# Sorted-order second mixture: x2, its logits and its dispatch kept in the order of the first mixture's groups

## The chip, the cores and the metric

The kernel runs on one core of a Trainium2 chip. The metric is the device time of one launch in microseconds (us).

## What is computed

Three stages follow each other. A linear-attention recurrence over 4 x 8 heads, 768 steps and 48 channels gives 3072 tokens of 384 numbers. The first mixture passes a token through one of 8 experts (384 to 1024 to 384) only if a score is positive; the others go on unchanged. The second, soft mixture needs all tokens: 32 slots are weighted sums over all tokens, 8 experts work on 4 slots each, and each token's output is a weighted sum of the 32 slot outputs.

```python
skip_score = x @ w_skip
do_compute = skip_score > 0
out = x.copy()
xc = x[do_compute]
logits = xc @ w_gate
e_idx = np.argmax(logits, axis=1)
...
for e in range(E):
    mask = e_idx == e
    h = np.maximum(xc[mask] @ w1[e], 0.0)
    y[mask] = gate_w[mask, None] * (h @ w2[e])
out[do_compute] = xc + y
...
logits = x @ phi
d = np.exp(logits - logits.max(0)); d /= d.sum(0) + 1e-09
slot_input = d.T @ x
...
c = np.exp(logits - logits.max(1)); c /= c.sum(1) + 1e-09
return c @ slot_out
```

## The kernel before

All five engines have their own hand-written instruction streams, joined by semaphores. P = 128 partitions; x is held as 24 tiles of 128 tokens x 384 (`x_sb`), all float32.

**Attention and gate** (up to about 165 us). 16 pairs of heads; then each tile is turned on TensorE (`gate_tiles`, L548), its scores are computed (`gate_scores`, L560) and turned back. The x tiles go to DRAM (`tokens`, L406), and zeros are written over `results` (L397).

**Routing front.** VectorE (L1116 to L1180) picks each token's expert, ranks the tokens with two products on TensorE (L603, L604), and builds one-hot tables. 24 narrow products (L611) invert them into lists: `take_i`, the token row for each place in sorted order, and `put_i`, where it goes back. TensorE runs filler products meanwhile (`idle_products`, L595: 8, 20, then 2 ahead of each of 8 register loads).

**First mixture.** The taken tokens stand sorted by expert, each expert padded to sub-tiles of 32; four sub-tiles are a group of 128 rows, and here there are 13 groups. GpSimd gathers the rows of a group with an indirect DMA (L1328) into `rows_in`. VectorE turns them (`turn_rows`, L1183); VectorE and ScalarE each copy half of a sub-tile's x (`take_x`, L1187 and L908); TensorE runs `first_layer` (L620) of the next sub-tile and then `second_layer` (L628) of this one; ScalarE applies relu (L917), VectorE turns the hidden values (L1194), ScalarE evicts the result (L936, L937) and VectorE adds its two halves (L1226). After four sub-tiles GpSimd scatters the 128 result rows to `results` (L1333). SyncE loads each next expert's weights as they come free, and the first slot experts' weights (L409 to L427).

**Collection.** When the last scatter has landed, SyncE reads `results` back in token order (L431). VectorE computes x2 = result x weight + x for 24 tiles (L1247), while TensorE turns them in six batches of four tiles (L690) and computes their logits (`slot_scores`, L672); 42 filler products (L670) stand ahead. The logits are exponentiated in two halves, each against its own maximum, turned, and used as dispatch weights (`dispatch`, L706); the halves are merged by rescaling (L1261 to L1272).

**Slot experts and output.** `slot_hidden` (L744) and `slot_back` (L759) run over 8 experts, whose weights SyncE loads into places as they come free (L433 to L447). Between them the comb weights (softmax over the slots) are turned (L777, L786) from logits that stayed in SBUF. After the fold (L792, L793) 24 output tiles are computed (L802), scaled by ScalarE and VectorE (L1006, L1292) and written in twelve DMAs (L451).

## Time and profile before

| | us |
|---|---|
| runs of the kernel | 400.13, 398.88, 398.15 (median 398.88) |
| the profiled execution | 398.49, clock granted on average 0.981 |
| its span, first to last instruction | 396.7 |
| busy: PE, weight load, DVE, ACT, POOL | 364.4, 278.1, 276.1, 219.6, 103.6 |
| data moved | 105.90 MB, mean 267 GB/s |

In the rows PE is TensorE, PEld its weight loads, DVE VectorE, ACT ScalarE, POOL GpSimd and SPq the queue of SyncE. A "x" counts instructions (a float32 product counts as two). In timelines an entry merges neighbouring instructions of one line; the bracket at its end is the idle time of the engine before it and what ended it. Times are from the span's start. PEclk is the granted TensorE clock as a share of 2.4 GHz.

### The profile page before, as it was taken

The numbers are of one execution on the slowest core, as the hardware profiler recorded it, in microseconds if no ns is written. First come the engines' busy times: TensorE is split into PE (matmuls) and PEld (weight loads), VectorE is DVE, ScalarE is ACT, GpSimd is POOL, SyncE is SP. The second block draws the span as 40 slices with busy tenths as digits, with TensorE's granted clock in tenths as the row PEclk, the third lists the DMA queues.
The fourth block names the chain that finished last, engine by engine and source line by source line (L and its number), as shares of the span: only waits on it lengthen the run. The fifth ranks groups of instructions, "written<-read, shape, count | busy, mean of one in ns | idle before, by whom it ended". The sixth has DMA issues, their size and how long they took to land.

```text
span 396.7 us, 14472 instructions
## 1 busy us (share of the span) xinstructions
PE 364.4 (92%) x5811; PEld 278.1 (70%) x5811; DVE 276.1 (70%) x557; ACT 219.6 (55%) x682; POOL 103.6 (26%) x136
## 2 busy tenths in 40 slices
PE   0799999999999999899999999999999999999980
PEld 0578877777777788787777777777777778855350
DVE  8999999999999934574666666666666654932051
ACT  1468777777677774304565565556565542841141
POOL 2222444334444360012322232222132330010000
PEclk9969999999999999999999999999999999999997
DMA  8956765567767999602195799696868817999839
GB/s 315 414 197 228 267 251 212 191 215 226 256 235 234 340 415 415 272 2 62 36 324 216 264 348 403 234 357 222 339 232 326 315 63 275 409 405 378 306 119 358
DMA packets 33432, 105.90 MB, mean 267 GB/s; under 512 B 3456, under 2 KB 14976, under 8 KB 31856
## 3 DMA queue, kind: packets, MB, share of 16 engines
q1 hardware_dynamic: 31536, 99.62, 67.7%
q0 software_dynamic: 1856, 5.70, 4.0%
q8 instruction: 30, 0.49, 0.5%
q14 instruction: 10, 0.08, 0.1%
HBM read 88.21 MB, written 17.10 MB: 265 GB/s over the span
## 4 chain that ended last, share of the span: by engine, by line
PE 55%; DVE 6%; DMA 2%; issue 1%; ACT 1%; SPq 0%; DVEq 0%; ACTq 0%; POOLq 0%
PE a_bank L624 18%; PE y_bank L633 17%; PE y_bank L749 3%; PE a_bank L765 3%; PE a_bank L557 2%; PE a_bank L690 2%; DVE x_sb L1292 1%; PE a_bank L597 1%; DMA back<-results 1%; PE y_bank L679 1%; PE y_bank L520 1%; PE a_bank L710 1%; DMA results<-work,put_now 1%; DVE k_in L1041 1%; PE y_bank L515 1%
## 5 line engine op out<-in xcount | busy, mean ns | idle before, releaser
L633 PE MATMUL y_bank<-w_sb,work 128*32 128x192 f32 x1664 | 78.5, 326 | 0.7 <-ACT work L937 0.7
L624 PE MATMUL a_bank<-w_sb,batch_t 128*32 128x256 f32 x1248 | 77.9, 381 | 0.0
L1315 POOL TENSOR_SCALAR_AFFINE_SELECT a_sb<-a_sb 128x512 f32<-128x512 f32 x48 | 51.3, 1071 | 85.6 <-ACT a_sb L837 85.6
L633 PEld LDWEIGHTS y_bank<-w_sb,work 128*32 128x32 f32 x1664 | 63.6, 110 | 10.8 <-DVE work L1194 3.4
L624 PEld LDWEIGHTS a_bank<-w_sb,batch_t 128*32 128x32 f32 x1248 | 42.2, 109 | 24.7 <-issue 11.0
L911 ACT ACTIVATE batch_t<-work 32x96 f32<-32x96 f32 x108 | 30.4, 281 | 45.3 <-PE a_bank L624 32.1
L1194 DVE STREAM_TRANSPOSE work<-hid 128x256 f32<-128x256 f32 x53 | 23.3, 440 | 35.2 <-PE y_bank L633 32.8
L847 ACT ACTIVATE bonus_v<-v_sb,bonus 128x48 f32<-128x48 f32 x192 | 44.9, 327 | 0.0
L494 PE MATMUL a_bank<-r_in,k_in 64*128 64x128 f32 x384 | 36.7, 313 | 1.2 <-DVE r_in L1042 0.3
L494 PEld LDWEIGHTS a_bank<-r_in,k_in 64*128 64x128 f32 x384 | 27.1, 200 | 11.5 <-issue 6.7
L1226 DVE TENSOR_TENSOR ys<-work 32x192 f32<-32x192 f32 x78 | 27.2, 348 | 8.7 <-ACT work L937 6.6
L936 ACT ACTIVATE work<-y_bank 64x192 f32<-64x192 f32 x52 | 16.8, 324 | 23.2 <-PE y_bank L633 22.9
L1019 DVE TENSOR_TENSOR_SCAN decay<-wrk_sb,ones_at 128x780 f32<-128x780 f32 x16 | 28.4, 1778 | 1.2
L1028 DVE TENSOR_TENSOR_SCAN decay<-wrk_sb,inv_at 128x780 f32<-128x780 f32 x16 | 28.7, 1795 | 0.1
L837 ACT ACTIVATE a_sb<-a_bank 128x512 f32<-128x512 f32 x48 | 28.4, 592 | 0.6 <-PE a_bank L494 0.6
L1189 DVE COPY batch_t<-work 32x96 f32<-32x96 f32 x108 | 26.4, 245 | 2.7 <-PE a_bank L624 0.4
L515 PE MATMUL y_bank<-r_in,state 64*48 64x128 f32 x320 | 21.4, 276 | 3.9 <-DVE x_sb L1055 3.9
L520 PE MATMUL y_bank<-a_sb,v_sb 128*48 128x128 f32 x384 | 24.3, 276 | 0.0
L1333 POOL DMA_INDIRECT results<-work,put_now x14 | 14.6, 1041 | 34.5 <-DVE work L1226 33.6
L515 PEld LDWEIGHTS y_bank<-r_in,state 64*48 64x48 f32 x320 | 18.2, 160 | 6.4 <-issue 5.9
L464 PE MATMUL ktok_bank<-ident,k_in 128*128 128x128 f32 x64 | 10.8, 293 | 12.9 <-DVE k_in L1041 12.9
L597 PE MATMUL a_bank<-ident 128*128 128x128 f32 x172 | 22.0, 290 | 0.4 <-DVE take_i L1170 0.3
(245 smaller groups left out, 569.2 us busy)
## 6 DMA issues: line engine op xcount, KB each, us to landing
w_sb<-in_moe_w SPq DMA_DIRECT2D x20, 1536.0 KB, 8.6
wrk_sb<-in_wrk SPq DMA_DIRECT2D x16, 768.0 KB, 7.6
e_sb<-in_moe_w SPq DMA_DIRECT2D x8, 1536.0 KB, 12.8
wrk_sb<-in_wrk SPq DMA_DIRECT2D x15, 780.0 KB
v_sb<-in_vt SPq DMA_DIRECT2D x16, 288.0 KB, 2.8
results<-work SPq DMA_DIRECT2D x1, 4608.0 KB, 15.2
tokens<-x_sb SPq DMA_DIRECT2D x4, 1152.0 KB, 23.0
x_sb<-in_moe_w SPq DMA_DIRECT2D x3, 1536.0 KB, 9.8
```

Of the source, the lines that this page charges most:

```text
L494: last = nc.tensor.matmul(a_bank[:, 2 * (g % 2) + a, (c % 2) * C:(c % 2 + 1) * C], k_in[rows, cols], r_in[n % 3][rows, cols], start=True, ...
L515: nc.tensor.matmul(y_cols[64 * a:64 * a + D, c * C:(c + 1) * C], state[n % 2][rows, :, c - 1], r_in[n % 3][rows, c * C:(c + 1) * C], start ...
L520: last = nc.tensor.matmul(y_cols[64 * a:64 * a + D, c * C:(c + 1) * C], v_sb[n % 4][:, c, a, :], a_sb[n % 2][:, a, c, :], start=False, sto ...
L624: last = nc.tensor.matmul(out[SUB * g:SUB * (g + 1), 0:FB], x[:, kk, :], w1_sb[j][:, kk, FB * g:FB * (g + 1)], start=(kk == 0), stop=(kk = ...
L633: last = nc.tensor.matmul(bank[4][SUB * g:SUB * (g + 1), 0:YW], h_t[:, SUB * k:SUB * (k + 1)], w2_sb[j][:, k, d:d + YW], start=(b == 0), s ...
L837: nc.scalar.activation(a_sb[n % 2][:, :, 2 * s:2 * s + 2, :].rearrange("p a c t -> p a (c t)"), a_bank[:, 2 * (g % 2):2 * (g % 2) + 2, 0:2 ...
L847: last = nc.scalar.activation(bonus_v[n % 2][:, c, a, :], v_sb[n % 4][:, c, a, :], ACT.Copy, scale=bonus[:, c, a:a + 1])
L911: last = nc.scalar.activation(x[SUB * o:SUB * (o + 1), :, :], turned[SUB * s:SUB * (s + 1), :].rearrange("p (k o t) -> p k o t", o=PER, t= ...
L1019: V.tensor_tensor_scan(decay[:, 0:SCAN], wrk_sb[i][:, 0:SCAN], ones_at[:, :], 0.0, ALU.mult, ALU.add).then_inc(mid_up_ready, 1)
L1028: V.tensor_tensor_scan(decay[:, SCAN:2 * SCAN], wrk_sb[i][:, SCAN:2 * SCAN], inv_at[:, :], 0.0, ALU.mult, ALU.add).then_inc(mid_down_ready, 1)
L1226: last = V.tensor_tensor(place_of[SUB * s:SUB * (s + 1), YW * d:YW * (d + 1)], y_low[rows, :], y_high[rows, :], ALU.add)
L1315: nc.gpsimd.affine_select(out=x, in_=x, compare_op=ALU.is_gt, fill=0.0, base=0, pattern=[[0, 2], [0, 2], [1, C]], channel_multiplier=-1).t ...
```

## The change

- `x_all` has 28 tiles, and `x_sb` is its last 24. The first mixture's result is no longer scattered: x2 of a group is made in SBUF, in sorted order, in `x_all[:, g]`. GpSimd copies the gathered rows there, gathers 128 gate weights from DRAM (`weights`), and adds the scaled results of the first 96 rows; VectorE adds the last 32.
- The tokens that skip the first mixture are dealt with ahead of the loop: phi logits of all 24 tiles come from the gate's turned tiles (six `gate_x` buffers instead of three), a mask product adds -1e30 for taken tokens, and all 24 tiles of `x_sb` are dispatched into bank 7 before the experts start.
- After the loop only the sorted tiles are turned: three batches of four, and a loop over the late batches, whose trip count is a register (at least 1; one for 13 groups). A mask from DRAM hides padding rows. Then 12 + 14 tiles are dispatched into two banks, and three parts are merged.
- Comb weights of the skipping tokens are stored to `combs[0]` in token order before the loop; those of sorted rows (32 numbers a row) are scattered by GpSimd to `combs[0]` and `combs[1]` in turn, and both are read back and added ahead of the last turn, which now stands behind the slot experts.
- All filler products go, and so do the fill of `results` with zeros over 4.6 MB (0.4 MB of `combs[1]` are cleared instead), the store and the reload of `results`. The slot experts' weights get other places and other waits.

The diff, cut to its core:

```diff
@@ SyncE @@
+            sp.wait_ge(weight_ready, 1)
+            with nc.allow_non_contiguous_dma(reason="a row of weights per partition"):
+                sp.dma_start(by_partition(weights), weight[:, :].unsqueeze(2)).then_inc(weight_stored, 16)
+            sp.wait_ge(mask_copied, 2)
+            sp.dma_start(masks, mask_bt).then_inc(tables_stored, 16)
+
+            sp.wait_ge(tables_stored, 16)
+            for i in range(BATCH):
+                sp.dma_start(mask_rows[NS * i:NS * (i + 1), :, :],
+                             masks.rearrange("(q i) t -> i q t", i=BATCH)[i:i + 1].to_broadcast([NS, XQ, P])).then_inc(ld_masks, 16)
+
+            sp.wait_ge(combs_a_ready, 1)
+            sp.dma_start(by_partition(combs[0])[:, 0:NT, :], comb[:, :, :]).then_inc(tables_stored, 16)
+
             sp.wait_ge(routed, 1)
-            groups = sp.value_load(tiles_i[0:1, E + 1:E + 2], min_val=1, max_val=MAX_GROUPS)
...
-            sp.wait_ge(results_stored, over)
-
-            for q in range(NT // 2):
-                sp.dma_start(back_rows(2 * q)[:, 2 * q % RING:2 * q % RING + 2, :],
-                             by_partition(results)[:, 2 * q:2 * q + 2, :]).then_inc(ld_rows[q], 16)
-            sp.wait_ge(x2_ready, RING)
+            sp.wait_ge(weigh_turned, 3)
+            load_e1(sp, 6)
+            sp.wait_ge(slot_parts_full, 2)
             load_e1(sp, 5)
-            sp.wait_ge(x2_ready, 2 * RING)
-            load_e1(sp, 4)
-            sp.wait_ge(x2_ready, NT)
-            load_e1(sp, 6)
-            sp.wait_ge(slot_parts_full, 1)
+            sp.wait_ge(slot_parts_full, 3)
             load_e1(sp, 7)
-            sp.wait_ge(slot_parts_full, 2)
             load_e2(sp, 4)
-            load_e2(sp, 5)
-            sp.wait_ge(slot_hidden_full, 1)
-            load_e2(sp, 6)
-            sp.wait_ge(slot_hidden_full, 2)
-            load_e2(sp, 7)
+            for e in range(5, E):
+                sp.wait_ge(slot_hidden_full, e - 4)
+                load_e2(sp, e)
+            sp.wait_ge(combs_all, 1)
+            for j, place in enumerate((comb[:, :, :], comb_odd)):
+                sp.dma_start(place, by_partition(combs[j])[:, 0:NT, :]).then_inc(ld_combs, 16)
...
@@ TensorE, front @@
+            for q in range(3):
+                phi_scores(q)
+            pe.wait_ge(pool_clear, 2)
+            nc.tensor.transpose(bank[7][0:NT, 3 * P:4 * P], mask_a[:, :], ident[:, :]).then_inc(mask_turned, 1)
+            phi_scores(3)
+            pe.wait_ge(mask_copied, 1)
+            for q in range(4):
+                mask_scores(q)
+            phi_scores(4)
+            phi_scores(5)
+            for q in range(4, NB):
+                mask_scores(q)
+            pe.wait_ge(logits_a_ready, 1)
+            turn(logit_t, logits_a_turned, 0, 4, bank[6])
+            pe.wait_ge(logits_a_ready, 2)
+            turn(logit_t, logits_a_turned, 4, NB, bank[4])
...
+            pe.wait_ge(weigh_ready, 1)
+            turn(weigh_t, weigh_turned, 0, 4, bank[0])
+            turn(weigh_t, weigh_turned, 4, NB, bank[1])
             pe.wait_ge(routed, 1)
+            pe.wait_ge(mask_b_ready, 1)
+            nc.tensor.transpose(bank[2][0:TILES, 0:P], mask_b[:, :], ident[:, :]).then_inc(mask_turned, 1)
             ends = [0]
+            pe.wait_ge(disp_ready, 1)
             for e in range(E):
-                idle_products(2)
+                n = NT * e // E
+                if n + NT // E > 16 >= n:
+                    pe.wait_ge(disp_ready, 2)
+                dispatch(n, n + NT // E, 0, NT, x_sb, bank[7])
                 ends.append(pe.value_load(tiles_i[0:1, e + 1:e + 2], min_val=1, max_val=MAX_GROUPS * PER))
+            pe.wait_ge(counts_ready, 2)
+            rest = pe.value_load(tiles_i[0:1, E + 2:E + 3], min_val=1, max_val=XQ - 3)
 
...
@@ TensorE, after the loop @@
+            x2_tiles(0)
+            x2_tiles(1)
+            early_scores(0)
+            x2_tiles(2)
+            early_scores(1)
+            pe.wait_ge(y_parts_ready, ends[E] + 1)
+            combs_turn(0, 0)
+            early_scores(2)
+            combs_turn(1, 1)
+            with pe.Fori(0, rest) as t:
+                pe.wait_ge(stage_ready, t + 1)
...
+                slot_scores(x_t4[1], bank[6], stage_turned)
+                pe.wait_ge(logit_t_ready, t + 4)
+                pe.wait_ge(combs_shifted, t + 2)
+                nc.tensor.transpose(bank[4][:, 3 * P:4 * P], logit_late[:, :], ident[:, :]).then_inc(combs_turned, 1)
+            pe.wait_ge(weigh_ready, 2)
+            turn(weigh_t, weigh_turned, 0, 3, bank[5])
+            pe.wait_ge(disp_ready, 3)
+            dispatch(0, 8, 0, B1, x_all, bank[0])
             pe.wait_ge(part_top_ready, 1)
-            nc.tensor.transpose(bank[0][0:1, 0:P], part_top[:, :], ident[:, :]).then_inc(tops_turned, 1)
-            pe.wait_ge(weigh_ready, 2)
-            turn(weigh_t, weigh_turned, HG, NB, bank[7])
-            dispatch(8, HG * BATCH)
+            nc.tensor.transpose(bank[2][0:1, 0:P], part_top[:, :], ident[:, :]).then_inc(tops_turned, 1)
+            combs_turn(2, rest + 2)
+            dispatch(8, B1, 0, B1, x_all, bank[0])
+            pe.wait_ge(weigh_ready, 3)
+            turn(weigh_t, weigh_turned, 3, XQ, bank[6])
             pe.wait_ge(top_row_ready, 1)
-            nc.tensor.matmul(bank[1][:, 0:1], top_row[:, :], ones[0:1, 0:1], start=True, stop=True).then_inc(tops_full, 1)
-            pe.wait_ge(disp_ready, 2)
-            dispatch(HG * BATCH, NT)
-
-            turn(logit_t, logits_turned, 0, 4, bank[6])
-            turn(logit_t, logits_turned, 4, NB, bank[7])
+            nc.tensor.matmul(bank[3][:, 0:1], top_row[:, :], ones[0:1, 0:1], start=True, stop=True).then_inc(tops_full, 1)
+            pe.wait_ge(disp_ready, 4)
+            dispatch(B1, MAX_GROUPS, B1, MAX_GROUPS, x_all, bank[1])
...
@@ VectorE, front @@
+            dve.wait_ge(logits_a_ready, 2)
+            V.tensor_reduce(less_part[:, 0:1], logit_t[:, 0:NB, :], AX.XY, ALU.max, negate=True).then_inc(less_a_ready, 1)
...
+            for j, n0, n1 in ((6, 0, 4 * BATCH), (4, 4 * BATCH, NT)):
+                dve.wait_ge(logits_a_turned, 1 if j == 6 else 2)
+                rows = bank[j][:, 0:(n1 - n0) * NS].rearrange("p (n s) -> p n s", s=NS)
+                link(V.tensor_reduce(top[:, n0:n1], rows, AX.X, ALU.max))
+                V.tensor_tensor(comb[:, n0:n1, :], rows, top[:, n0:n1].unsqueeze(2).to_broadcast([P, n1 - n0, NS]),
+                                ALU.subtract).then_inc(combs_a_shifted, 1)
...
@@ VectorE, end of a group @@
+                late = slice(TOK - SUB, TOK)
+                x2 = x_all[late, bass.ds(g, 1), :].rearrange("p o d -> p (o d)")
+                dve.wait_ge(ys_added, PER * g + PER + 1)
+                dve.wait_ge(ld_weight, 16 * g + 16)
+                dve.wait_ge(rows_kept, g + 1)
+                V.scalar_tensor_tensor(out=x2, in0=ys[late, :], scalar=weight_now[late, :], in1=x2,
+                                       op0=ALU.mult, op1=ALU.add).then_inc(x2_done, 1)
...
@@ VectorE, after the loop @@
+            dve.wait_ge(ld_masks, 64)
+            copy_tiles(0)
+            copy_tiles(1)
+            logits_of(0)
+            copy_tiles(2)
+            logits_of(1)
+            shift_combs(0, 1)
+            link(logits_of(2))
+            V.tensor_reduce(less_part[:, 1:2], group_top[:, 1:4], AX.X, ALU.max, negate=True).then_inc(less_part_ready, 1)
+            shift_combs(1, 2)
+            with dve.Fori(0, rest) as t:
...
+            dve.wait_ge(ld_combs, 32)
+            V.tensor_tensor(comb[:, :, :], comb[:, :, :], comb_odd, ALU.add).then_inc(combs_added, 1)
...
@@ ScalarE, after the loop @@
+            for q in range(3):
+                copy_tiles(q)
+            for q in range(2):
+                comb_exps(q, q + 1)
+            weigh(1, 0, 3)
+            with act.Fori(0, rest) as t:
+                for i in range(0, BATCH, 2):
+                    act.wait_ge(x2_transposed, BATCH * t + 3 * BATCH + i + 1)
+                    nc.scalar.activation(x_t4[1][:, :, i, :], bank[i][:, 0:DM].rearrange("p (k t) -> p k t", t=P),
+                                         ACT.Copy).then_inc(x2_copied_act, 1)
+                act.wait_ge(combs_shifted, t + 3)
+                nc.scalar.activation(comb_rows[:, bass.ds(t + 3, 1), :], comb_rows[:, bass.ds(t + 3, 1), :], ACT.Exp).then_inc(combs_ready, 1)
+            copy_disp(3, 0, 3 * BATCH, bank[5])
+            weigh(2, 3, XQ)
...
@@ GpSimd @@
+            with pool.Fori(0, groups) as g:
+                wait(x2_done, g + 1)
+                nc.gpsimd.tensor_copy(weight_i[:, :], put_i[:, bass.ds(g, 1)]).then_inc(index_ready, 1)
+                wait(index_ready, 2 * g + 1)
+                take_weights(weight_i[:, :])
+                wait(ld_rows_in, 16 * g + 32)
+                nc.gpsimd.tensor_copy(x_all[:, bass.ds(g + 1, 1), :].rearrange("p o d -> p (o d)"), rows_in).then_inc(rows_kept, 1)
+                nc.gpsimd.tensor_copy(take_now[:, :], put_i[:, bass.ds(g + 2, 1)]).then_inc(index_ready, 1)
+                wait(rows_turned, g + 2)
+                wait(rows_kept, g + 2)
+                wait(index_ready, 2 * g + 2)
+                take_rows(take_now[:, :])
+                wait(ld_weight, 16 * g + 16)
+                wait(ys_added, PER * g + PER)
+                x2 = x_all[:, bass.ds(g, 1), :].rearrange("p o d -> p (o d)")
+                early = slice(0, TOK - SUB)
+                nc.gpsimd.tensor_scalar(scaled[early, :], ys[early, :], weight_now[early, :], None, ALU.mult).then_inc(ys_taken, 1)
+                wait(ys_taken, g + 2)
+                nc.gpsimd.tensor_tensor(x2[early, :], scaled[early, :], x2[early, :], ALU.add).then_inc(x2_early, 1)
+            wait(x2_done, groups + 1)
+            wait(x2_early, groups)
+            wait(ld_rows_in, 16 * groups + 32)
+            pool.sem_inc(x2_done, 3 * BATCH)
+            pool.sem_inc(x2_early, 3 * BATCH)
+            pool.sem_inc(x2_all, 1)
+            with pool.Fori(0, rest) as t:
+                wait(stage_turned, t + 1)
+                for i in range(BATCH):
+                    last = nc.gpsimd.tensor_copy(stage[:, i, :], x_all[:, bass.ds(BATCH * t + 3 * BATCH + i, 1), :].rearrange("p o d -> p (o d)"))
+                last.then_inc(stage_ready, 1)
...
+            for q in range(3):
+                if q < 2:
+                    pool.wait_ge(combs_ready, q + 1)
+                else:
+                    wait(combs_ready, rest + 3)
+                for i in range(BATCH):
+                    g = BATCH * q + i
+                    if g >= 2:
+                        pool.wait_ge(combs_stored[g % 2], 16 * (g // 2))
+                    put_combs(put_i[:, g:g + 1], comb_rows[:, q, NS * i:NS * (i + 1)], g % 2)
+            with pool.Fori(0, late_groups) as g:
+                wait(combs_stored[0], 16 * g + 16 * 6)
...
+                wait(index_ready, 2 * groups + g + 1)
+                put_combs(put_now[:, :], late_rows, 0)
+            wait(combs_stored[0], 16 * late_groups + 16 * 6)
+            pool.wait_ge(combs_stored[1], 16 * 6)
+            pool.sem_inc(combs_all, 1)
 
 
```

## Rows read from the trace of the kernel before

**Rows 1.** The page: busy time, share of the span and instructions of each engine.
```profile
PE 364.4 (92%) x5811; PEld 278.1 (70%) x5811; DVE 276.1 (70%) x557; ACT 219.6 (55%) x682; POOL 103.6 (26%) x136
```
**Rows 2.** Stretches of the kernel: length, each engine's busy time, PEclk, DMA share, GB/s.
```profile
164.90:181.65 16.75, 14.87 (x116) 13.70 (x114) 12.42 (x46) 1.22 (x5) 1.72 (x4) 0.90 0.07 24
181.65:323.65 142.00, 141.27 (x2915) 106.02 (x2914) 89.78 (x272) 83.03 (x260) 40.20 (x67) 1.00 0.71 260
323.65:355.06 31.41, 30.55 (x367) 23.69 (x364) 18.49 (x45) 15.08 (x40) 1.78 (x2) 1.00 0.84 318
355.06:379.20 24.14, 23.86 (x338) 11.97 (x338) 3.56 (x7) 4.02 (x11) 1.84 (x2) 1.00 0.88 315
379.20:396.70 17.50, 7.17 (x52) 4.90 (x52) 7.37 (x14) 6.09 (x13) 0.00 (x0) 0.86 0.69 270
```
**Rows 3.** Timeline of the routing front: start, duration, instruction, idle time before it.
```profile
175.60 0.19 DVE L1170 TENSOR_SCALAR take_i<-y_bank 128x28 uint32<-128x28 f32 x1 [0.36 <-PE y_bank L611]
...
176.71 5.01 PE L597 MATMUL a_bank<-ident 128*128 128x128 f32 x28 [0.15 <-issue]
176.77 1.21 POOL L1323 DMA_INDIRECT parts<-tokens,take_i  x1 [28.14 <-DVE take_i L1170]
...
180.13 0.58 DVE L1185 STREAM_TRANSPOSE work<-parts 128x384 f32<-128x384 f32 x1 [2.73 <-DMA parts<-tokens,take_i]
...
181.65 0.64 PE L624 MATMUL a_bank<-w_sb,batch_t 128*32 128x256 f32 x8
```
**Rows 4.** Stretches of the routing front, columns as in rows 2.
```profile
173.47:176.88 3.41, 2.98 (x29) 2.62 (x30) 2.88 (x14) 0.00 (x0) 0.11 (x1) 1.00 0.02 5
176.88:180.29 3.41, 3.41 (x17) 3.41 (x17) 0.64 (x3) 0.00 (x0) 1.48 (x3) 0.50 0.19 58
```
**Rows 5.** Timeline of the experts' loop around the end of a group.
```profile
298.19 1.06 POOL L1328 DMA_INDIRECT parts<-tokens,take_now  x1 [0.86 <-POOL take_now L1361]
...
302.60 0.50 POOL L1367 COPY work<-ys 96x384 f32<-96x384 f32 x1
303.02 0.72 DVE L1226 TENSOR_TENSOR work<-work 32x192 f32<-32x192 f32 x2 [0.27 <-ACT work L937]
...
303.77 0.50 DVE L1189 COPY batch_t<-work 32x96 f32<-32x96 f32 x2
304.22 0.38 ACT L917 ACTIVATE hid<-a_bank 128x256 f32<-128x256 f32 x1
...
304.72 1.05 PEld L624 LDWEIGHTS a_bank<-w_sb,batch_t 128*32 128x32 f32 x24 [0.23 <-issue]
...
305.21 0.45 DVE L1194 STREAM_TRANSPOSE work<-hid 128x256 f32<-128x256 f32 x1 [0.94 <-PE y_bank L633]
...
307.44 0.58 DVE L1185 STREAM_TRANSPOSE work<-parts 128x384 f32<-128x384 f32 x1 [0.20 <-DVE batch_t L1189]
```
**Rows 6.** All instructions of a line: duration min/median/max in ns, first and last start.
```profile
L1247 DVE SCALAR_TENSOR_TENSOR x_sb<-w_sb,weight,x_sb x16: 608/612/617, 337.0 to 345.8; 128x384 f32<-128x384 f32 x16
...
L1041 DVE TENSOR_TENSOR k_in<-wrk_sb,decay x16: 946/1386/1393, 10.1 to 136.3; 128x768 f32<-128x768 f32 x16
```
**Rows 7.** Timeline after the experts' loop.
```profile
324.56 0.71 DVE L1226 TENSOR_TENSOR work<-work 32x192 f32<-32x192 f32 x2 [0.27 <-ACT work L937]
...
332.10 2.20 DVE L1247 SCALAR_TENSOR_TENSOR x_sb<-back,weight,x_sb 128x384 f32<-128x384 f32 x4 [6.13 <-DMA back<-results]
...
338.46 1.53 PE L690 MATMUL a_bank<-ident,x_sb 128*128 128x128 f32 x12
...
339.92 0.86 PE L679 MATMUL y_bank<-work,phi_sb 128*32 128x128 f32 x24
...
352.09 2.14 PE L710 MATMUL a_bank<-x_sb,disp 128*32 128x384 f32 x24
...
352.72 0.62 DVE L1268 TENSOR_SCALAR parts<-a_bank,rescale 128x384 f32<-128x384 f32 x1 [0.36 <-ACT rescale L973]
...
356.29 4.09 PE L749 MATMUL y_bank<-e_sb,batch_t 128*32 128x256 f32 x72 [0.20 <-ACT batch_t L981]
...
359.23 0.95 DVE L1282 TENSOR_REDUCE norm<-comb 128x24 f32<-128x768 f32 x1 [0.91 <-ACT comb L984]
...
379.20 0.62 DVE L1286 TENSOR_SCALAR parts<-a_bank,slot_norm 128x384 f32<-128x384 f32 x1 [18.47 <-PE a_bank L765]
```
**Rows 8.** A stretch of the slot experts' weight loads, columns as in rows 2.
```profile
331.00:375.40 44.40, 43.33 (x594) 27.01 (x596) 20.27 (x47) 18.45 (x48) 2.58 (x3) 1.00 1.03 385
```

More of the change, by code:

```diff
@@ L29, in build @@
     NB = B * NC // BATCH
-    RING = 8
+    BIG = 1e30
     E, F = w1.shape[0], w1.shape[2]
@@ L89, in build @@
         tokens = nc.dram_tensor("tokens", [P * LINE, DM], F32).ap()
-        results = nc.dram_tensor("results", [P * LINE, DM], F32).ap()
+        weights = nc.dram_tensor("weights", [P * LINE, 1], F32).ap()
+        masks = nc.dram_tensor("masks", [TILES, P], F32).ap()
+        combs = [nc.dram_tensor(f"combs{j}", [P * LINE, NS], F32).ap() for j in range(2)]
         logit = sb("logit", [P, NT, E + 1])
```

524 lines of the change are left out of this document (305 added, 219 removed).

## The prediction, written before the changed kernel ran

> **What bounds the kernel now.** I first read the share of busy time: TensorE (PE) is busy 92% of the span [rows 1]. That is an average, so next I cut the span at the stage borders [rows 2]. Up to 164.9 us lies the attention with the gate, which the change barely touches. The routing front takes 16.75 us, the experts' loop 142.00 us (PE 141.27 busy: nothing else sets its length), the stretch from the last expert product to the slot inputs 31.41 us, the slot experts 24.14 us, the output 17.50 us. So in the loop any delay of PE is lost one for one, and elsewhere the waits between the engines decide. In the front the order is: indices at 175.79, gather issued 176.77, its rows turned from 180.13 on, while PE runs filler products from 176.71 to 181.72 and starts on the experts at 181.65 [rows 3]. Both chains end together there. In the third stretch 8.5 us pass between the last sum (from 324.56) and the first x2 tile (332.10 and one operation on), most of it the store and reload of the results [rows 7].
>
> **The sum's base.** It goes against the profiled execution, 398.49 us (span 396.7); the median of the runs is 398.88, so 0.4 above. A measurement of this kernel tells about 0.5%, 2 us, from no change.
>
> **Front: +3.8 us.** Added on PE are the phi scores (6 groups as large as the x2 scores of 0.86 us [rows 7]), mask scores and turned logits; they take the place of 8 + 20 filler products and fit before the one-hot tables of VectorE (DVE), which still pace the 24 rank products, so they cost nothing. If they were late, they would push the indices by what they are late. Added on DVE before take_i is one maximum over 768 columns, 0.95 us by the reduction of that size [rows 7], of which 0.7 fall into an idle gap: +0.3. Behind the indices PE now has, in place of filler, 6 turned weight tiles (1.0 us), the mask turn (0.3) and the dispatch of all 24 token tiles. Twelve tiles take 24 products at 2.14 us with the tail [rows 7], so 24 take 3.9 us at full clock. They also wait for the maximum, an exponential over 768 columns on ScalarE (ACT, about 1.0 us) and ACT's copy (0.6): indices 176.1, exponential until 177.0, turned 178.2, copied and started at 178.9. With the eight register loads between them, which the filler shows at no more than 0.6 us a step (5.01 / 8) [rows 3], the eight steps need 5 us at full clock: 184.0, and 0.4 for one more register. The clock adds: it was granted at 0.50 (1.2 GHz) from 176.88 to 180.29, behind the stretch in which PE ran mostly the narrow rank products [rows 4]. In the new order less dense work follows that stretch, so I let the dispatch run at 1.2 GHz for 1.5 to 5 us, +0.5 to +2 us. PE is ready at 184.8 to 187; I take 185.5 against 181.7. The lower end is that only the gather chain counts: DVE has 2.2 us of comb logits and a register more before it turns the rows, done 1.3 us later than now. Bounds +1.3 and +5.5.
>
> **Loop: +6.5 us.** Per group of four sub-tiles (13 groups, one every 10.8 us) the store of 128 result rows goes, and DVE gets one multiply-add (x2 of the last 32 rows, 384 columns) between its sum at sub-tile 3 and its copy of the next x. Is there room? The sum ran 303.02 to 303.74, the copy 303.77 to 304.27 without a gap, and PE's next first layer began to load weights at 304.72; it was not DVE but ACT's relu, ending at 304.60, that released it 0.12 later [rows 5]. With the same 0.12 DVE has 0.33 us of room. The multiply-add costs 0.61 us over 384 columns [rows 6] (on 128 partitions; for 32 I take the same), and the three waits on registers in front of it about the 0.20 us that the turn of the gathered rows sat idle behind three such waits [rows 5]. 0.81 - 0.33 = 0.48 us of PE lost at each of 12 borders: 5.8 us. GpSimd (POOL) now also does a copy, a scaling and an addition per group where it did one copy of 0.50 us [rows 5]. DVE's product with two SBUF inputs took 0.95 or 1.39 us [rows 6], the longer value where POOL was masking; I charge 0.06 of these 0.44 us at each border, since the two meet only in part: 0.7 us over the loop. Bounds: 0, if the room is larger than read, and +10, if each border loses 0.8. I take 6.5, nearest to the row of the border.
>
> The Trainium skill (GPSIMD Reference, Key points) says that GpSimd shares its SBUF interfaces with VectorE and contends with instructions that have two SBUF inputs. The rows with 0.95 and 1.39 us agree with it; by that rule alone each border would lose another 0.28 us (0.61 x 0.46), 3.4 us in the loop instead of 0.7.
>
> **POOL's queue in the loop**: the gather of the rows two groups ahead now stands behind the weight gather, its wait and the copy into x_all. Two gathers at 1.06, three small operations and three big ones, with 0.86 of idle before an issue [rows 5], make about 8 us; the period is 10.8, and the rows are needed 10 us after their issue. So nothing, unless the list is 3 us longer (a rival).
>
> **After the last product: -3.9 us.** T is the end of the last second layer, 323.73. Gone are 42 filler products, the store, the reload and 24 multiply-adds. x2 is there, so PE turns tiles from T on. Three batches of 4 tiles: in the kernel before a batch is 1.53 + 0.86 = 2.3 us of PE [rows 7]. Now DVE evicts two tiles a batch (0.62 each from PSUM [rows 7]), adds the mask and takes the maximum (0.3 each, an estimate between the 0.16 of one column and the 0.62 of 384), and it is first busy with its last sum, the multiply-add and the fold table (324.56 is T + 0.8; 0.71, 0.81 and 0.8) until T + 3.1: the three batches end at T + 9.1. The loop over the late batches runs once (13 groups) and serially: turn 1.5, ACT's copies behind two exponentials, scores 0.8, mask, maximum, turn back, row maximum, until T + 15. The tail (turned weights, 12 + 14 = 26 tiles of dispatch at 0.17, where the kernel before has 24, exponentials, the merge of three parts) adds 10.8, with the slot inputs: slot products start at T + 26.5 instead of 356.29 = T + 32.6. That is 6.1 us sooner. The two turns of the comb leave the slot stage (0.8 us of PE) for the gap in which PE waits for DVE. PE would be done at T + 48.4, where now DVE's last scaling starts at 379.20 = T + 55.5.
>
> But the comb weights must come back first. Weights of slot experts load until 375.4 at 385 GB/s, 4.2 us for each 1.57 MB [rows 8]. In the new order only one is loaded early; SyncE issues four more after T + 24.2, and one still runs: the queue is busy until T + 46. The comb reload (0.79 MB, 2.1 us) is issued behind them by SyncE and lands about T + 48.9. Then DVE adds, sums over 768 columns (0.95 each [rows 7]) and inverts, 2.7 us, and only then scales: T + 51.6. Gain 55.5 - 51.6 = 3.9 us. Bounds: 6.9 if the reload lands early, 1.5 if the late batch runs at 1.2 GHz. POOL's 13 scatters of 128 bytes a row, in two alternating chains of about 3 us a link, end near T + 36, so they hide behind the weight loads; without that cover each further microsecond a link costs 6.
>
> The Trainium skill (DMA: Bandwidth & Descriptors, Queues, rings and completion order) says that each DMA engine takes turns between queues packet by packet. By it the scatters don't stand behind the weights, while the reload, on SyncE's own queue, does.
>
> The output (17.50 us) and the start are unchanged; the zero fill of 4.6 MB that goes was waited for by nobody.
>
> **Sum:** 398.5 + 3.8 + 6.5 - 3.9 = 404.9; I say 405.
>
> **The rivals.** (a) Forecast: work taken off the end is paid for in front and at PE's borders, 402 to 409. Chance 0.50. For it: PE has no idle time in the loop [rows 2]. (b) The other side: the multiply-add fits into the room of DVE, and the reload lands in time. The price of the loop is 0, the end gives 6.1 + 0.8 = 6.9, the front costs 1.3 to 3.8: 393 to 395.5. It decides if DVE's added step is below 0.33 us or the next first layer can start later than the row shows without loss. For it speaks that DVE is idle 0.94 us behind that copy [rows 5]. Chance 0.22. (c) The parts cancel: loop 3, front 3, end -5.5, 399. Chance 0.15. (d) POOL becomes the bound of the loop: its list per group reaches 11.8 us instead of 8, each group waits 1 us: +12 on a sum without the border stalls, about 411. It decides from a list of 10.8 us on. Against it: the rows add up to less. Chance 0.13. The change does what it says only if sorted tiles need no second pass over unsorted rows; the diff leaves none.
>
> **How the numbers follow.** Slower by over 0.5%: (a) and (d), 0.63. Same: (c), 0.15. Faster: (b), 0.22. The range leaves out the faster half of (b) and the slower half of (d): 395 to 411. The likeliest case alone is 402 to 409.
>
> **What would show it.** In the changed trace: the first layer starts near 185.5, not 181.7; the loop's stretch is near 148.5 us, with PE waiting for DVE's x copy once a group and POOL's last addition done before the next multiply-add; the first slot product comes 26 to 28 us after the last second layer; DVE's wait before the comb addition ends on the reload. A loop of 142 us would prove the border stall wrong, one of 154 would point to POOL; a comb addition that DVE starts long before the last slot product would prove the queue argument wrong.

## The result: 418.65 us, and the profile after

The changed kernel takes 418.65 us (median of 4 runs, 416.59 to 419.95) against 398.51 (median of 4, 397.85 to 400.13): 1.0494 times the time, 95% interval 1.044 to 1.0548, where I had forecast 405 (395 to 411). The sign was right; the size was not, and the range did not hold it. The profiled execution took 419.95 us (span 417.8). Below, lines of its page: busy times, the granted clock in 40 slices, the loop's first-layer products, and the sums of the loop.

```profile
PE 362.5 (87%) x5824; PEld 268.0 (64%) x5824; DVE 293.3 (70%) x578; ACT 215.6 (52%) x670; POOL 148.6 (36%) x183
PEclk9969999999999999989999999999999998899757
L728 PE MATMUL a_bank<-w_sb,batch_t 128*32 128x256 f32 x1248 | 78.4, 382 | 11.2 <-DVE batch_t L1328 10.4
L1366 DVE TENSOR_TENSOR ys<-work 32x192 f32<-32x192 f32 x104 | 44.2, 425 | 8.1 <-ACT work L1064 7.3
```

TensorE's work is the same as before within 2 us [rows 1]; what is new stands behind the bar of its first-layer row: 10.4 us of idle time until DVE's copy of the next x (`batch_t`, L1328). Cut at the same stage borders as [rows 2] (front, loop, loop's end to slot inputs, slot experts, output; columns as there):

```profile
164.90:185.85 20.95, 17.92 (x282) 11.08 (x282) 15.78 (x53) 5.89 (x15) 5.93 (x11) 0.92 0.17 53
185.85:340.00 154.15, 143.26 (x2915) 108.51 (x2916) 105.36 (x283) 82.89 (x259) 68.05 (x91) 1.00 0.62 226
340.00:371.40 31.40, 24.37 (x278) 14.78 (x282) 17.74 (x48) 8.21 (x22) 11.96 (x15) 0.89 0.48 174
371.40:399.10 27.70, 21.56 (x274) 9.59 (x266) 2.41 (x5) 1.73 (x6) 4.66 (x7) 0.88 0.78 279
399.10:417.80 18.70, 9.13 (x53) 6.35 (x52) 7.35 (x14) 6.84 (x15) 0.00 (x0) 0.68 0.65 253
```

The third and fourth borders lie elsewhere in the work than before, so I compare by events, with T the end of the last second layer (323.73 before, 339.98 after):

| | before | after | change | forecast |
|---|---|---|---|---|
| start to first expert product | 181.65 | 185.87 | +4.2 | +3.8 |
| loop, to T | 142.08 | 154.11 | +12.0 | +6.5 |
| T to first slot product | 32.56 | 28.18 | -4.4 | -6.1 |
| T to DVE's last scaling | 55.47 | 59.02 | +3.6 | -3.9 |
| last scaling to the end | 17.5 | 18.8 | +1.3 | 0 |

The first, second and last two rows add up to the 21.1 us between the spans 396.7 and 417.8.

**The loop.** One border between two groups in the changed kernel (timeline: start, duration, engine, instruction, idle time before it):

```profile
291.81 1.25 POOL L1571 TENSOR_SCALAR free_rows<-ys,weight_now 96x384 f32<-96x384 f32 x1 [2.17 <-DVE ys L1366]
...
293.31 1.00 POOL L1573 TENSOR_TENSOR x_all<-free_rows,x_all 96x384 f32 x1 [0.26 <-POOL free_rows L1571]
293.65 1.24 DVE L1366 TENSOR_TENSOR ys<-work 32x192 f32<-32x192 f32 x2 [0.18 <-ACT work L1064]
...
295.21 0.62 DVE L1373 SCALAR_TENSOR_TENSOR x_all<-ys,weight_now,x_all 32x384 f32 x1 [0.32 <-DVE ys L1366]
...
295.86 0.50 DVE L1328 COPY batch_t<-work 32x96 f32<-32x96 f32 x2
...
296.46 1.50 PE L728 MATMUL a_bank<-w_sb,batch_t 128*32 128x256 f32 x24 [0.87 <-DVE batch_t L1328]
```

Three things differ from [rows 5]. The pair of sums takes 1.24 us instead of 0.72 while POOL's addition runs. Behind it come 0.32 us of wait (0.20 forecast) and 0.62 of multiply-add (0.61 forecast). And TensorE starts 0.87 us late.

**The end.** POOL's scatters of the comb weights, from 352.64 on (seven of thirteen), and then what waits for them:

```profile
354.03 0.99 POOL L1515 DMA_INDIRECT combs<-free_rows,put_i  x1 [0.31 <-issue]
...
358.63 0.97 POOL L1515 DMA_INDIRECT combs<-free_rows,put_i  x1 [0.72 <-issue]
363.50 0.97 POOL L1515 DMA_INDIRECT combs<-free_rows,put_i  x1 [3.90 <-DMA combs<-free_rows,put_i]
...
369.57 0.97 POOL L1515 DMA_INDIRECT combs<-free_rows,put_i  x1 [3.82 <-DMA combs<-free_rows,put_i]
...
376.83 0.97 POOL L1515 DMA_INDIRECT combs<-free_rows,put_i  x1 [5.02 <-DMA combs<-free_rows,put_i]
...
383.66 0.97 POOL L1515 DMA_INDIRECT combs<-free_rows,put_i  x1 [4.59 <-DMA combs<-free_rows,put_i]
...
385.84 0.99 POOL L1515 DMA_INDIRECT combs<-logit,put_now  x1 [0.86 <-POOL logit L1600]
```
```profile
369.73 10.71 SPq L401 DMA_DIRECT2D e_sb<-in_moe_w  x3
...
391.81 0.34 SPq L493 DMA_DIRECT2D comb<-combs  x1
392.20 0.43 SPq L493 DMA_DIRECT2D free_rows<-combs  x1
392.23 2.47 PE L881 MATMUL a_bank<-e_sb,batch_t 128*32 128x384 f32 x16 [2.53 <-DMA e_sb<-in_moe_w]
...
396.58 0.96 DVE L1459 TENSOR_TENSOR comb<-comb,free_rows 128x768 f32<-128x768 f32 x1 [27.42 <-DMA free_rows<-combs]
...
399.00 0.52 DVE L1465 TENSOR_SCALAR parts<-a_bank,slot_norm 128x384 f32<-128x384 f32 x1
```

The chain of scatters ends at T + 51.8 instead of T + 36; only then is the reload issued. Median time from issue to landing, in the stretch up to 358 us without weight traffic, and in the stretch 358 to 395 at 321 GB/s:

```profile
combs<-free_rows,put_i POOLq DMA_INDIRECT x4, 2.2
```
```profile
combs<-free_rows,put_i POOLq DMA_INDIRECT x8, 5.7
```

### The profile page after: what moved, and what is told of

Same layout as the page of the kernel before. It is cut to its first block, busy times and chain, and to the rows that moved or that the text cites. A ratio compares the mean times of both kernels' runs of the same rounds, so it can differ in the third digit from the quotient of the medians.

```text
span 417.8 us, 14718 instructions
## 1 busy us (share of the span) xinstructions
PE 362.5 (87%) x5824; PEld 268.0 (64%) x5824; DVE 293.3 (70%) x578; ACT 215.6 (52%) x670; POOL 148.6 (36%) x183
## 4 chain that ended last, share of the span: by engine, by line
PE 36%; DVE 12%; DMA 8%; issue 6%; ACT 3%; POOL 1%; DVEq 1%; ACTq 0%; POOLq 0%; SPq 0%
PE a_bank L728 14%; PE y_bank L737 13%; DMA combs<-free_rows,put_i 5%; DVE ys L1366 4%; PE a_bank L602 2%; DVE batch_t L1328 1%; DMA combs<-logit,put_now 1%; PE sums_bank L674 1%; ACT work L1064 1%; POOL combs L1515 1%; DMA free_rows<-combs 1%; DVE x_all L1471 1%; PE a_bank L784 1%; PE a_bank L918 1%; DVE k_in L1166 1%
## 5 line engine op out<-in xcount | busy, mean ns | idle before, releaser
L728 PE MATMUL a_bank<-w_sb,batch_t 128*32 128x256 f32 x1248 | 78.4, 382 | 11.2 <-DVE batch_t L1328 10.4
L737 PEld LDWEIGHTS y_bank<-w_sb,work 128*32 128x32 f32 x1664 | 65.7, 110 | 8.3 <-DVE work L1333 0.8
L1366 DVE TENSOR_TENSOR ys<-work 32x192 f32<-32x192 f32 x104 | 44.2, 425 | 8.1 <-ACT work L1064 7.3
L539 PEld LDWEIGHTS a_bank<-r_in,k_in 64*128 64x128 f32 x384 | 27.2, 200 | 11.7 <-issue 6.7
L1328 DVE COPY batch_t<-work 32x96 f32<-32x96 f32 x108 | 26.5, 246 | 9.5 <-PE a_bank L728 6.8
L1571 POOL TENSOR_SCALAR free_rows<-ys,weight_now 96x384 f32<-96x384 f32 x13 | 16.2, 1247 | 26.8 <-DVE ys L1366 24.4
L1505 POOL DMA_INDIRECT parts<-tokens,take_now x13 | 15.1, 1158 | 23.3 <-issue 17.1
L1042 ACT ACTIVATE hid<-a_bank 128x256 f32<-128x256 f32 x53 | 20.4, 384 | 5.1 <-PE a_bank L728 3.8
```

Source lines behind the costliest of these rows:

```text
L539: last = nc.tensor.matmul(a_bank[:, 2 * (g % 2) + a, (c % 2) * C:(c % 2 + 1) * C], k_in[rows, cols], r_in[n % 3][rows, cols], start=True, ...
L728: last = nc.tensor.matmul(out[SUB * g:SUB * (g + 1), 0:FB], x[:, kk, :], w1_sb[j][:, kk, FB * g:FB * (g + 1)], start=(kk == 0), stop=(kk = ...
L737: last = nc.tensor.matmul(bank[4][SUB * g:SUB * (g + 1), 0:YW], h_t[:, SUB * k:SUB * (k + 1)], w2_sb[j][:, k, d:d + YW], start=(b == 0), s ...
L1328: last = V.tensor_copy(x[SUB * o:SUB * (o + 1), :, :], turned[SUB * s:SUB * (s + 1), :].rearrange("p (k o t) -> p k o t", o=PER, t=SUB)[:, ...
L1366: last = V.tensor_tensor(ys[SUB * s:SUB * (s + 1), YW * d:YW * (d + 1)], y_low[rows, :], y_high[rows, :], ALU.add)
```

## The experiments

All derive from the changed kernel; T is the end of the last second layer in each. e1, e2, e3, e5, e6 and a0 were run once, with a profile; the others were timed in 4 runs (e10 in 6). Times that end in a stage are from the profiled execution.

### The border: which of the two engines costs

**e1** (e1_no_pool_math): GpSimd's arithmetic left out.
```
- nc.gpsimd.tensor_scalar(scaled[early, :], ys[early, :], weight_now[early, :], ...).then_inc(ys_taken, 1)
- nc.gpsimd.tensor_tensor(x2[early, :], scaled[early, :], x2[early, :], ALU.add).then_inc(x2_early, 1)
+ pool.sem_inc(ys_taken, 1)
+ pool.sem_inc(x2_early, 1)
```


> GpSimd's scaling and addition of rows 0 to 95 in each group are left out (those rows of x2 are wrong in the output); VectorE's multiply-add of the last 32 rows, with its waits, stays. Theory A (the two engines slow each other: VectorE's sum in sub-tile 3 takes 1.24 us a pair beside GpSimd's addition, 0.72 elsewhere): the pair is back near 0.72, a border costs about 0.5 us less, and the stage of the groups is 154.1 - 12 x 0.5 = about 148 us. Theory B (VectorE's own added work at the border, 0.32 of wait and 0.62 of multiply-add, is the whole cost, since 0.94 x 12 = 11.3): the stage stays at 153 to 154.

Measured: 411.85 us, loop 147.71 (186.14 to 333.85), so 6.4 less. Its page row has the sum at a mean of 359 ns:
```profile
L1366 DVE TENSOR_TENSOR ys<-work 32x192 f32<-32x192 f32 x104 | 37.3, 359 | 9.5 <-ACT work L1064 7.5
```
Theory A's number.

**e2** (e2_no_dve_step): VectorE's multiply-add of the last 32 rows and its waits left out.
```
- V.scalar_tensor_tensor(out=x2, in0=ys[late, :], scalar=weight_now[late, :], in1=x2, ...).then_inc(x2_done, 1)
+ dve.sem_inc(x2_done, 1)
```


> VectorE's multiply-add of the last 32 rows and its waits are left out (those rows of x2 are wrong in the output); GpSimd's scaling and addition stay. Theory A: what is left is the slow pair of sums, 0.52 us later in each border, less what slack the next sub-tile has: 144 to 148 us for the stage of the groups. Theory B: the stage is back at 142 to 142.5.

Measured: 407.24 us, loop 143.06. The sums are still slow beside POOL (timeline, 303 to 309 us, and the page's mean):
```profile
307.27 1.00 POOL L1569 TENSOR_TENSOR x_all<-free_rows,x_all 96x384 f32 x1 [0.26 <-POOL free_rows L1567]
307.56 1.30 DVE L1366 TENSOR_TENSOR ys<-work 32x192 f32<-32x192 f32 x2 [0.18 <-ACT work L1064]
```
```profile
L1366 DVE TENSOR_TENSOR ys<-work 32x192 f32<-32x192 f32 x104 | 46.2, 444 | 10.9 <-ACT work L1064 9.4
```
Neither theory had it quite: the 0.6 us of slow sums (1.30 for 0.71) are there and cost next to nothing, since the border has about that much room when DVE has nothing else to do.

**e3** (e3_neither): both left out.

> Both steps are left out (all rows of x2 wrong in the output), so that the loop does only what it did before. Both theories: 142.0 us for the stage of the groups, 11.83 a group back to 10.83. If it stays above 143, something else that the change put into the loop (the gather of weights, its index) costs, and neither theory is enough.

Measured: 409.13 us, loop 142.40; all else in the loop costs 0.3 us over the kernel before. (The whole is longer than e2 because its first expert product came 2.5 us later, at 187.65, of which 2.4 us stand ahead of the front (first phi product at 167.19 against 164.82).) The four loops side by side, above 142.4 and per border (12): POOL's arithmetic alone 0.7 us (0.05), DVE's step alone 5.3 (0.44), both 11.7 (0.98). The parts don't add: whichever comes second finds the room used up.

**e4** (e4_step_in_gap): one multiply-add of all 128 rows on DVE, in the idle time of the next group's sub-tile 0; POOL without arithmetic.
```
+ def x2_step(g):
+     x2 = x_all[:, bass.ds(nc.s_assert_within(g - 1, 0, TILES - 3), 1), :].rearrange("p o d -> p (o d)")
+     dve.wait_ge(ys_added, PER * g + 1)
...
+     V.scalar_tensor_tensor(out=x2, in0=ys[:, :], scalar=weight_now[:, :], in1=x2, ...).then_inc(x2_done, 1)
...
  take_x((s + 2) % PER)
...
+ if step and s == 0:
+     x2_step(g)
  dve.wait_ge(h_ready, PER * g + s + 2)
```


> The whole computation. One multiply-add of all 128 rows on VectorE, in sub-tile 0 of the next group between its take of the next hidden rows and its turn of the hidden layer, where it idles 0.94 us a group; GpSimd does no arithmetic in the loop. Theory A: both parts of the cost go, the multiply-add (0.6 to 0.7 us) fits the idle time: stage of the groups 142 to 143.5, whole 407 to 409 us. Theory B (VectorE's added work is what costs, wherever it is): 0.6 x 12 = 7 stay, stage 149, whole 414.

Measured: 407.01 us (median of 4), 1.02 times the kernel before, interval 1.0128 to 1.0271; loop 142.41. The multiply-add lies where DVE idled 0.94 us [rows 5], for four times the rows in the same 0.62 us:
```profile
308.13 0.50 DVE L1325 COPY batch_t<-work 32x96 f32<-32x96 f32 x2
308.67 0.62 DVE L1347 SCALAR_TENSOR_TENSOR x_all<-ys,weight_now,x_all 128x384 f32 x1
309.45 0.45 DVE L1330 STREAM_TRANSPOSE work<-hid 128x256 f32<-128x256 f32 x1 [0.17 <-PE y_bank L735]
```
Theory A. The whole loss of the loop is gone, and 8.6 us over the kernel before remain, so the end and the front must hold them.

### The end: scatters, weights and the queue

**e5** (e5_no_scatter): the 13 scatters left out (`put_combs` and their waits; the wait for the last exponential stays).

> The 13 scatters of the comb weights are left out (the comb part of the output is wrong); the reload, the weight loads and everything else stay. Theory A (the chain of scatters is what delays DVE's last scaling, which starts 59.1 us after T, T being the end of the last second layer): the reload is issued right behind the last weights, and the last slot product, T + 54.8 in the changed kernel, decides: scaling at T + 55.3, some 4 us sooner. Theory B (the weights of the slot experts, five of which load after T + 22, are the bound just behind it and are themselves slowed by the scatters): the last weight lands sooner too and the scaling starts at T + 52 or before.

Measured: 420.83 us. The whole is no guide, for its loop took 159.7 us (below). Against its own T (345.71) the scaling starts at T + 55.5, 3.5 us sooner:
```profile
comb<-combs SPq DMA_DIRECT2D x1, 384.0 KB, 11.1
free_rows<-combs SPq DMA_DIRECT2D x1, 384.0 KB, 9.6
```
```profile
396.88 1.50 PE L881 MATMUL a_bank<-e_sb,batch_t 128*32 128x384 f32 x16 [2.60 <-DMA e_sb<-in_moe_w]
```
```profile
398.76 0.96 DVE L1459 TENSOR_TENSOR comb<-comb,free_rows 128x768 f32<-128x768 f32 x1 [25.57 <-DMA free_rows<-combs]
```
The time was theory A's, but not for its reason. The changed kernel itself scaled at T + 57.4 when it was run again (a0), so the scatters account for 2.0 to 3.5 us. The reload is now issued at T + 39 (384.97), and lands 9.6 to 11.1 us later, where it took 3.7 and 4.4 in the changed kernel. It stands behind the weights of its own queue; the last of these arrives at T + 51.2. With the scatters that was T + 52.2, and T + 50.1 in a0, so it isn't shown that the scatters slow the weights. Behind the scatters the weights are waiting as the next bound, and they are 5 us later than the T + 46 of my forecast.

**e6** (e6_no_late_weights): the seven late weight loads and TensorE's waits for them left out, old data used.
```
- load_e1(sp, 6)
...
- load_e1(sp, 7)
- load_e2(sp, 4)
- for e in range(5, E):
-     sp.wait_ge(slot_hidden_full, e - 4)
-     load_e2(sp, e)
```


> The loads of the late slot weights (first layers 5 to 7, second layers 4 to 7) are left out and old data is used in their place (slot part of the output wrong); the 13 scatters stay. Theory A (a scatter of 128 rows of 128 bytes lands in 5 to 6 us only because it shares the DMA engines with weights; idle it took 2.1): the links of the two chains shorten to 3 to 3.5 us, the reload is issued before T + 42, and the slot products run without a gap to T + 50.3: scaling at T + 50.5. Theory B (the small rows themselves need 5 to 6 us): the chain still ends near T + 51.5 and the scaling is as late as in the changed kernel, T + 57 or later.

Measured: 414.97 us (loop again slow, 159.4). T is 344.66; the reload's addition comes at T + 42.0, the scaling at T + 50.5 right behind slot products without a gap:
```profile
386.64 0.96 DVE L1449 TENSOR_TENSOR comb<-comb,free_rows 128x768 f32<-128x768 f32 x1 [12.64 <-DMA free_rows<-combs]
...
395.17 0.62 DVE L1455 TENSOR_SCALAR parts<-a_bank,slot_norm 128x384 f32<-128x384 f32 x1 [6.03 <-PE a_bank L871]
```
Theory A: the scatters are slow because weights travel beside them. Where the scatters of a chain wait for each other they now start 2.9 to 4.1 us apart, under weights 6.1 to 7.3, and the reload is issued at T + 37.6, close to the T + 36 of the forecast.

**e9** (e9_gap_three): e4 with three comb tables, so three chains of scatters; SyncE reloads.
```
- combs = [nc.dram_tensor(f"combs{j}", ...).ap() for j in range(2)]
+ combs = [nc.dram_tensor(f"combs{j}", ...).ap() for j in range(3)]
...
- if g >= 2:
-     pool.wait_ge(combs_stored[g % 2], 16 * (g // 2))
+ if g >= 3:
+     pool.wait_ge(combs_stored[g % 3], 16 * (g // 3))
```


> The whole computation: the multiply-add in the gap as in the run e4_step_in_gap (407.0 us; comb addition at T + 57.1), and three comb tables in DRAM in place of two, so that three chains of scatters run beside each other. SyncE still issues the reload. Theory A (the chain of scatters alone is late): the scatters are over by T + 44, and the comb addition starts near T + 50. Theory B (the reload, on SyncE's own queue, stands behind the weights that it has issued, the last of which land at T + 55.2): three loads of 0.7 us each of share behind them, addition at T + 57 to 58, no gain: 406 to 408 us.

Measured: 410.93 us, 1.0317 times before (1.0285 to 1.035), about 4 us slower than e4 by the medians. The profiled execution was the fastest of the four, 407.72 us, and no slower than that of e4 (408.47), so the trace doesn't hold the 4 us. In it the reload is issued at 372.28, T + 44.7, as theory A had it, and the addition starts at T + 55.7, as theory B had it:
```profile
comb<-combs SPq DMA_DIRECT2D x1, 384.0 KB, 8.1
free_rows<-combs SPq DMA_DIRECT2D x1, 384.0 KB, 8.7
disp<-combs SPq DMA_DIRECT2D x1, 384.0 KB, 10.1
```
The last weights release TensorE at 380.43, and none of the three loads has landed before 380.3.

**e10** (e10_gap_three_pool): as e9, but POOL issues the reload (`sp.dma_start` becomes `nc.gpsimd.dma_start`, behind a wait for the last dispatch).

> The whole computation, as e9_gap_three, but GpSimd issues the reload on its own queue, beside the weights of SyncE. Theory B: the reload lands near T + 48 to 50, takes about 2 us from the weights, and the last slot product (T + 55.5 to 57.5) decides: scaling T + 56 to 58 in place of 59.5, whole 404 to 406 us. Theory A: same as e9_gap_three.

Measured: 410.03 us, 1.025 times before (1.0211 to 1.029). Both expectations missed: issued at T + 47.5 the three loads still need 6.8 to 8.3 us, and they take their share from the weights, of which one now needs 20.2 us to land (at most 16.4 in e9). The addition starts at T + 57.0, the scaling at T + 62.9. The slot products had begun only at T + 32.3. What the trace shows is two late starts while POOL issues eight scatters back to back (339.75 to 348.46). DVE's mask addition, whose product had ended at 341.1, starts at 343.66, and ACT's copy of turned weights, which had been turned by 345.2, starts only at 348.41. Behind that TensorE ran at half clock (0.50 from 345 to 350):
```profile
343.66 0.29 DVE L1422 TENSOR_TENSOR parts<-ktok_bank,free_rows 128x128 f32<-128x128 f32 x1 [3.86 <-remote]
...
348.41 0.49 ACT L1019 ACTIVATE disp<-y_bank 128x384 f32<-128x384 f32 x1 [2.74 <-remote]
```
e9 shows the late addition (4.5 us of idle time) but not the late copy. With waits between the scatters the addition started 0.3 us behind its product. What holds the two engines was not tried apart.

### What is left to gain

**a0** (a0_after_again): the changed kernel, unedited.

> The changed kernel once more, unedited. In the runs e5_no_scatter and e6_no_late_weights the stage of the groups took 159.7 and 159.4 us, though their edits lie wholly behind it; the changed kernel took 154.1. If that stage has two paces that come and go from run to run, this one can show 154 or 159.5; if the pace belongs to the program, 154.1 again and 417 to 420 us for the whole.

Measured: 420.14 us, loop 154.16 again. So the changed kernel has one pace, and the slower one was seen only in e5 and e6, once each. Whether it belongs to these programs or to their executions isn't shown. It shows as 0.4 us more at sub-tile 1 of each group, where DVE and ACT start together on x. Why stays open. This run shows another thing, by its stretch from T to the first slot product beside that of the first profile (clock in the third column from the right):
```profile
341.80:368.30 26.50, 19.50 (x218) 11.74 (x218) 16.77 (x46) 8.21 (x22) 10.43 (x13) 0.94 0.46 163
```
```profile
340.00:368.10 28.10, 21.13 (x218) 12.80 (x218) 16.72 (x46) 8.20 (x22) 10.44 (x13) 0.88 0.42 153
```
Same instructions, 1.6 us apart: here the slot products start at T + 26.6, the forecast's 26.5. The rest of the 28.2 is half clock (1.2 GHz). The first expert product came later here, at 187.59. 1.7 us of that lie ahead of the front, and the dispatch took 6.42 us for 5.75, at a lower clock (0.55 against 0.91 from 180 to 185.5).

**e11** (e11_gap_order): e4, with DVE's scaling and TensorE's fold of the slot outputs moved ahead of the comb addition (a swap of the two blocks on each engine).

> The whole computation: as e4_step_in_gap (407.0 us), and in the end VectorE scales the slot outputs and TensorE folds them before they turn to the comb weights, where the changed kernel does it behind the comb addition and its sums (0.96, 0.95, 0.18, 0.30 us). Theory A (the chain of scatters and the reload set the end, so only what stands behind the reload counts): scaling at the end of the last slot product, T + 55.5, and the first output product 2 to 3 us sooner than in e4_step_in_gap: 404 to 405 us. Theory B (the weights set the end): no more than 1 us, 406.

Measured: 406.65 us, 1.017 times before (1.0096 to 1.0244). The scaling moved from T + 59.5 to T + 56.2, but the addition came at T + 58.8, 1.7 us later than in e4, and the first output product at T + 62.1, as in e4 (T + 62.2):
```profile
384.27 0.62 DVE L1464 TENSOR_SCALAR parts<-a_bank,slot_norm 128x384 f32<-128x384 f32 x1 [25.92 <-PE a_bank L878]
386.62 0.36 DVE L1466 COPY ys<-a_bank 128x192 f32<-128x192 f32 x1 [1.74 <-PE a_bank L902]
386.90 0.95 DVE L1468 TENSOR_TENSOR comb<-comb,free_rows 128x768 f32<-128x768 f32 x1
```
The reload was issued at 381.34 and needed 3.8 us, so it had landed by 385.2 (T + 57.1). What delayed the addition is what now stands ahead of it: the scaling, 1.74 us of waiting for the fold, which ran at half clock, and the copy. The swap thus undid its own gain: 0.4 us at most (the runs spread by more). That is theory B's size, but its reason, the weights, isn't shown by it. The addition ahead of the wait for the fold was not tried.

**e12** (e12_gap_order_fill): e11 with fillers.
```
+ def fill(count):
+     for _ in range(count):
+         nc.tensor.matmul(bank[5][:, 0:P], ident[:, :], ident[:, :], start=True, stop=True)
  for e in range(EH, E):
+     if e >= E - 2:
+         fill(14)
      slot_back(e)
```


> The whole computation: as e11_gap_order, with 28 products of filler (14 ahead of each of the last two slot products, where TensorE waits for weights) and 6 more where it waits for the comb weights. If the half clock granted during the output (1.2 GHz from 392.6 us on in the changed kernel) comes from TensorE having stood idle just before, the output runs at 2.4 GHz and the whole is 1 to 1.5 us shorter than e11_gap_order; if not, it is the same or 1 us longer.

Measured: 405.81 us, 1.0163 times before (1.013 to 1.0197). TensorE ran at 2.4 GHz from 350 us up to the output products (clock 1.00), and the profiled span is 403.8. The slots began at T + 26.5, but that isn't the fillers' work: they stand behind it (from 373.94). The output products themselves ran at 2.4 GHz until 394, as expected if idle time causes the half clock; only behind them did the clock fall, to a mean of 0.74 over the stretch:
```profile
388.40:403.80 15.40, 6.25 (x48) 4.29 (x48) 6.39 (x12) 5.77 (x12) 0.00 (x0) 0.74 0.79 308
```
The same stretch took 16.3 us in e11, at 0.60, so full clock was worth 0.9 us there. The medians are 0.8 us apart, less than the spread of the runs; 1 to 1.5 was expected.

**e13** (e13_gap_order_fill_front): e12, four of the register loads moved ahead of the dispatch in front.

> The whole computation: as e12_gap_order_fill, with four of the eight register loads of the experts' ends taken out of the dispatch of the first tiles and put where TensorE waits for the weights ahead of it. If the dispatch is paced by the loads (0.65 us a step, 5.75 for eight steps, where 48 products alone need about 4.3 us at full and more at half clock), the first layer starts 1 to 2 us sooner (184 to 184.8 instead of 185.5); if it is paced by the half clock alone, no sooner.

Measured: 405.79 us, 1.0176 times before (1.0122 to 1.023). First layer at 186.12, no sooner. The two loads put ahead of the turns, with the wait that goes before them, made these late (2.69 us of idle time where 1.32 were). The dispatch took 5.4 us instead of 5.8 though its clock was lower (0.67 against 0.92 from 180 to 185.5). So the loads paced the dispatch at least in part, and what moving them saved there was lost ahead of the turns; which part of that is the wait was not tried.

## Why the forecast's sign was right and its size wrong

**Front, forecast +3.8, measured +4.2: right.** Start 185.87 for 185.5; the dispatch ran at 5.75 us for eight steps, partly at half clock, as described. Two other executions (a0, e3) started at 187.6, 1.7 us of it from ahead of the front.

**Loop, forecast +6.5, measured +12.0: the term for POOL beside DVE was mis-sized.** The step charged 0.06 us a border because "the two meet only in part". They meet at every border: POOL's addition (293.31 to 294.31) covers the first 0.66 us of DVE's last sums, and the pair takes 1.24 us for 0.72. e1 prices it at 6.4 us (154.11 - 147.71) instead of 0.7. The own step of DVE was forecast at 5.8 us and e1 against e3 measures 5.3. That is close in part by luck: wait and multiply-add were 0.94 us for the 0.81 forecast, and with a cost of 0.44 the room was 0.50, not 0.33. The two costs don't add: e2 shows that the contention alone is nearly free (0.7 us); it costs in full only because DVE's step has used the room. The Trainium skill (SBUF — State Buffer, Who interferes with whom) says that a VectorE instruction with two SBUF inputs contends with a GpSimd instruction that reads SBUF. The trace agrees: both inputs of the sum are in SBUF, and 0.35 us becomes 0.88 here and at most 1.07. By the rule I had set 3.4 us beside the sum; the multiply-add that I applied it to was never slowed (616 to 619 ns in all 13), since POOL's addition had ended before it; the sums ahead of it were.

**T to the slot products, forecast -6.1, measured -4.4: right at full clock** (a0, e1, e5, e12, e13: T + 26.4 to 26.6). The bound "1.5 if the late batch runs at 1.2 GHz" covers what happened.

**T to the last scaling, forecast -3.9, measured +3.6: two terms failed.** "About 3 us a link, ending near T + 36" held only without weights (2.9 to 4.1 us, e6). Under weights a link took 6.1 to 7.3 us, because a scatter then lands after 5.7 us instead of 2.2, and the chains ended at T + 51.8; e6 shows that the weights make the difference. The warning stood in the text ("without that cover each further microsecond a link costs 6") but not in the range. And "the queue is busy until T + 46" was T + 52.2 (T + 51.2 without scatters, e5): six weight loads start from T + 22 on, where I counted one running at T + 24 and four behind it, and the last is issued only at 376.0 (T + 36) and lands 16.1 us later. From 369.73 on the queue issues the last three without a gap, at 2.3 to 4.4 us each where the first took 0.37; why an issue takes that long stays open. With that bound alone the end would have gained nothing: T + 55.5 in e5, as before. That the reload stands behind the weights of its queue was right (e5, e9; in e10, on POOL's queue, it landed ahead of the last weights). The Trainium skill (DMA: Bandwidth & Descriptors, Queues, rings and completion order) has the engines take turns between queues by packets; that agrees with the scatters landing at all among the weights, yet the turn costs them 3.5 us each, which I had read as free.

**Output, forecast 0, measured +1.3.** TensorE had waited for the reload, and the clock granted in the output was 0.68, where it was 0.86 [rows 2]. With 0.84 and 0.85, in e5 and e6, the output took 17.5 and 17.6 us; with 0.68 in a0 again 18.8.

The four errors, 0.4 + 5.5 + 7.5 + 1.3 = 14.7 us, make up the distance from 405 to the profiled 419.95 but for 0.2. Rival (d) gave 411 for a loop 12 us longer; its size was right, its cause (POOL's list as the bound) was not: e2 runs POOL's whole list in 143.06 us. My sign "one of 154 would point to POOL" was thus half right: POOL was the cause through DVE's sums, not through its list. Rival (b) fell with the room: e4 shows that the room exists, one sub-tile later. With the loop mended (e12) 7.1 us stay between the spans (403.8 and 396.7): 4.1 in front, 0.3 in the loop, 2.7 behind T. No version here beats the kernel before.

## What to carry to other kernels

Price an added step by the sum of everything that newly meets at its place, and compare that sum with the room once. Here the slowed sums (0.5 to 0.6 us) alone cost 0.05 a border, DVE's step (0.9) alone 0.44, both together 0.98, against a room of about 0.5. Look for the idle time on the same engine a few operations on before you split a step over two engines. A chain of small transfers must be priced by its landing time under the traffic that will run beside it, and a stage that ends sooner must be checked for what its transfers wait on.
